# Eight buffers in place of four for the input chunks in the front of a spectral mix and FFN kernel

## What is computed

```python
X = np.fft.rfft(x, axis=1)
Yr = X.real @ w_r - X.imag @ w_i + b_r
Yi = X.real @ w_i + X.imag @ w_r + b_i
Y = soft(Yr, 0.01) + 1j * soft(Yi, 0.01)     # sign(y) * max(|y| - lam, 0)
y = np.fft.irfft(Y, n=3008, axis=1)
h = y.reshape(-1, 256) @ w_in
g = (a0 + a1*h + a2*h**2 + a3*h**3) / (1 + |b0|*|h| + |b1|*h**2 + 1e-6)
out = g @ w_out
```

## Time and profile before

| | us |
|---|---|
| median of 3 runs | 1433.96 |
| lowest and highest | 1433.38, 1437.82 |
| the profiled execution | 1435.4 |
| its span in the trace | 1433.5 |
| TensorE busy in the span | 1384.9 (97%) |
| VectorE | 1332.4 (93%) |
| ScalarE | 1249.6 (87%) |
| GpSimd | 632.1 (44%) |

### The profile page before, as it was taken

One profiled execution on the slowest core, in us unless ns is written; L12 is line 12 of the kernel. 1 busy time (PEld: TensorE's weight loads), 2 busy tenths in 40 slices (PEclk: granted clock), 3 DMA queues, 4 the chain that ended last, 5 costly groups with the idle time before them and its releaser, 6 DMA issues.

```text
span 1433.5 us, 21592 instructions
## 1 busy us (share of the span) xinstructions
PE 1384.9 (97%) x7498; PEld 972.4 (68%) x7498; DVE 1332.4 (93%) x1639; ACT 1249.6 (87%) x1654; POOL 632.1 (44%) x417
## 2 busy tenths in 40 slices
PE   7998999999999999999999999999999999999987
PEld 3775677667766677676777776776766666666666
DVE  6587989989999999999999999999999999999998
ACT  4577999988889989988989989988889999999986
POOL 0001544435444444444445444444545555555554
PEclk9999999999999999999999999999999999999999
DMA  8976756656556655555455555565445546555443
GB/s 275 293 230 140 173 129 140 154 129 140 119 130 137 143 135 131 126 115 122 105 130 114 130 108 129 110 133 115 94 103 113 117 82 122 108 114 111 85 94 70
DMA packets 97913, 188.07 MB, mean 131 GB/s; under 512 B 11216, under 2 KB 57744, under 8 KB 97808
## 3 DMA queue, kind: packets, MB, share of 16 engines
q0 software_dynamic: 29952, 98.58, 37.1%
q1 hardware_dynamic: 67856, 88.12, 20.7%
HBM read 50.60 MB, written 37.49 MB: 61 GB/s over the span
## 4 chain that ended last, share of the span: by engine, by line
PE 54%; DVE 18%; ACT 16%; issue 8%; DMA 3%; POOL 1%; SPq 0%; ACTq 0%; POOLq 0%
PE h_ps L564 19%; PE o_ps L594 7%; PE o_ps L579 6%; PE o_ps L581 6%; DVE den L1092 4%; DVE num L1098 4%; DVE g_hi L1087 4%; DVE num L1112 4%; PE d L541 3%; ACT num L794 3%; ACT sq L791 3%; ACT den L788 3%; ACT sq L857 3%; PE d L505 2%; DMA spec<-s_out 2%
## 5 line engine op out<-in xcount | busy, mean ns | idle before, releaser
L1175 POOL TENSOR_TENSOR g_lo<-num,sq 128x940 fp32r<-128x940 f32 (+1 forms) x205 | 468.8, 2287 | 97.6 <-DVE num L1098 97.0
L1167 POOL DMA_DIRECT2D den<-sq x208 | 182.5, 877 | 690.7 <-ACT sq L791 367.3
L579 PE MATMUL o_ps<-g_hi,wout_hi 128*128 128x470 f32 (+1 forms) x832 | 342.9, 413 | 2.2 <-DVE g_hi L1087 2.2
L581 PE MATMUL o_ps<-g_hi,wout_lo 128*128 128x470 f32 (+1 forms) x832 | 310.9, 374 | 0.0
L564 PE MATMUL h_ps<-yt_hi,win_hi 128*128 128x470 f16 (+1 forms) x832 | 300.8, 362 | 4.6 <-DVE num L1115 4.6
L564 PE MATMUL h_ps<-yt_lo,win_hi 128*128 128x470 f16 (+1 forms) x832 | 298.7, 359 | 0.0
L564 PE MATMUL h_ps<-yt_hi,win_lo 128*128 128x470 f16 (+1 forms) x832 | 298.7, 359 | 0.0
L1112 DVE TENSOR_TENSOR num<-h_ps,num 128x940 f32<-128x940 f32 (+1 forms) x208 | 232.3, 1117 | 31.4 <-ACT num L794 30.7
L1115 DVE SCALAR_TENSOR_TENSOR num<-num,coef,h_ps 128x940 f32<-128x940 f32 (+1 forms) x208 | 245.1, 1179 | 7.4
L1098 DVE SCALAR_TENSOR_TENSOR num<-num,a_sb,den 128x940 f32<-128x940 f32 (+1 forms) x208 | 244.4, 1175 | 0.1
L1087 DVE SCALAR_TENSOR_TENSOR g_hi<-num,a_sb,sq 128x940 fp32r<-128x940 f32 (+1 forms) x208 | 244.4, 1175 | 0.0
(11 more groups left out here) (167 smaller groups left out, 1571.7 us busy)
## 6 DMA issues: line engine op xcount, KB each, us to landing
den<-sq POOLq DMA_DIRECT2D x200, 470.0 KB, 4.4
z_in<-spec SPq DMA_DIRECT2D x96, 128.0 KB, 2.5
spec<-s_out SPq DMA_DIRECT2D x96, 128.0 KB, 1.9
xw<-in_x SPq DMA_DIRECT2D x31, 384.0 KB, 4.9
out_t<-o_sb SPq DMA_DIRECT2D x25, 470.0 KB, 4.5
spec<-s1w SPq DMA_DIRECT2D x56, 192.0 KB, 2.9
zp_in<-spec SPq DMA_DIRECT2D x22, 480.0 KB, 5.6
inv_in<-in_inv SPq DMA_DIRECT2D x96, 64.0 KB, 2.3
```

The source lines that it names most:

```text
L579: pe.matmul(o_ps[:, h, 0:w], wout_hi[:, f, h * P:(h + 1) * P], g_hi[q % 3][:, j, 0:w], start=f == 0, stop=False)
L581: mm = pe.matmul(o_ps[:, h, 0:w], wout_lo[:, f, h * P:(h + 1) * P], g_hi[q % 3][:, j, 0:w], start=False, stop=False)
L1175: pool.tensor_tensor(g_lo[r % 2][:, :, 0:cols(r)], ring(num, r), ring(sq, r), ALU.mult).then_inc(n_g, 1)
```

## The change

The chunks of x get eight buffers in the front. The four new ones are the first 96 partitions of the four num tiles. A new function x_place gives the buffer of chunk k: k % 8 for k < 10, and k % 4 from then on; x_loads counts how often a buffer was loaded, for the waits. SyncE issues chunks 4 to 7 directly after the bias, without a wait, and chunks 8 and 9 after the stores of g = 11 and g = 13 (before: 9 and 11). The load of the first four weight parts, which use num, gets two waits on all of batch 0's steps. Each buffer has its semaphore, so s_x has eight.

```diff
+def x_place(k):
+
+    return k % 8 if k < S1N // 2 + 2 else k % 4
+
+
+def x_loads(k):
+
+    return sum(1 for u in range(k + 1) if x_place(u) == x_place(k))
+
...
+        x_in += [num[i][0:ROWS, :].rearrange("r (p d) -> r p d", d=D) for i in range(4)]
...
-        s_x = [sem(f"s_x{i}") for i in range(4)]
+        s_x = [sem(f"s_x{i}") for i in range(8)]
...
             def load_x(k):
-                if k >= 4:
-                    sp.wait_ge(p1, 2 * (k - 3))
-                    if k - 3 <= FRONT_S1 // 2:
-                        sp.wait_ge(x_dve, 2 * (k - 3))
-                    else:
-                        sp.wait_ge(x_dve, FRONT_S1)
-                        sp.wait_ge(x_act, 2 * (k - 3) - FRONT_S1)
+                user = [u for u in range(k) if x_place(u) == x_place(k)]
+                if user:
+                    sp.wait_ge(p1, 2 * user[-1] + 2)
+                    sp.wait_ge(x_dve, min(2 * user[-1] + 2, FRONT_S1))
+                    if 2 * user[-1] + 2 > FRONT_S1:
+                        sp.wait_ge(x_act, 2 * user[-1] + 2 - FRONT_S1)
                 n, chunk = divmod(k, S1N // 2)
...
                 if i < 4:
+                    sp.wait_ge(p1, S1N)
+                    sp.wait_ge(x_dve, S1N)
...
-            for k in range(1, 4):
+            for k in range(1, 8):
                 load_x(k)
-            load(mix_stage(0), w_r.rearrange("(h p) e -> p h e", p=P), s_wc)
-            load(mix_stage(1), w_i.rearrange("(h p) e -> p h e", p=P), s_wc)
-            load(bias_sb[:, :], bias, s_wc)
+                if k == 3:
+                    load(mix_stage(0), w_r.rearrange("(h p) e -> p h e", p=P), s_wc)
+                    load(mix_stage(1), w_i.rearrange("(h p) e -> p h e", p=P), s_wc)
+                    load(bias_sb[:, :], bias, s_wc)
             for g in range(S1N):
                 store_s1(g)
-                if g % 2 == 1 and g // 2 + 4 < S1N // 2 + 2:
-                    load_x(g // 2 + 4)
+                if g % 2 == 1 and g // 2 + 3 in (S1N // 2, S1N // 2 + 1):
+                    load_x(g // 2 + 3)
...
-                    pe.wait_ge(s_x[g // 2 % 4], (g // 8 + 1) * 16)
+                    pe.wait_ge(s_x[x_place(g // 2)], 16 * x_loads(g // 2))
```

More of the change, by code:

```diff
@@ L325, in load_x @@
             def load_x(k):
-                if k >= 4:
-                    sp.wait_ge(p1, 2 * (k - 3))
-                    if k - 3 <= FRONT_S1 // 2:
-                        sp.wait_ge(x_dve, 2 * (k - 3))
-                    else:
-                        sp.wait_ge(x_dve, FRONT_S1)
-                        sp.wait_ge(x_act, 2 * (k - 3) - FRONT_S1)
+                user = [u for u in range(k) if x_place(u) == x_place(k)]
[4 more added lines that the diff above has]
+                        sp.wait_ge(x_act, 2 * user[-1] + 2 - FRONT_S1)
                 n, chunk = divmod(k, S1N // 2)
-                load(x_in[k % 4].rearrange("r p d -> r (p d)"), x[n, :, chunk * 4 * D:(chunk + 1) * 4 * D], s_x[k % 4])
+                load(x_in[x_place(k)].rearrange("r p d -> r (p d)"), x[n, :, chunk * 4 * D:(chunk + 1) * 4 * D], s_x[x_place(k)])
             def load_z(c):
@@ L472, in step_s1 @@
                 else:
-                    pe.wait_ge(s_x[g // 2 % 4], (g // 8 + 1) * 16)
+                    pe.wait_ge(s_x[x_place(g // 2)], 16 * x_loads(g // 2))
                 at = g % 2 * 2
-                pe.matmul(bank[0:ROWS], c1_sb[:, :], x_in[g // 2 % 4][:, at:at + 2, :].rearrange("r p d -> r (p d)"),
+                pe.matmul(bank[0:ROWS], c1_sb[:, :], x_in[x_place(g // 2)][:, at:at + 2, :].rearrange("r p d -> r (p d)"),
                           start=True, stop=True).then_inc(p1, 1)
@@ L737, in sum_abs @@
             def sum_abs(g):
-                act.wait_ge(s_x[g // 2 % 4], (g // 8 + 1) * 16)
+                act.wait_ge(s_x[x_place(g // 2)], 16 * x_loads(g // 2))
                 if g > FRONT_S1:
@@ L741, in sum_abs @@
                 at = g % 2 * 2
-                act.activation(x_size[0:ROWS, :], x_in[g // 2 % 4][:, at:at + 2, :].rearrange("r p d -> r (p d)"), ACT.Abs,
+                act.activation(x_size[0:ROWS, :], x_in[x_place(g // 2)][:, at:at + 2, :].rearrange("r p d -> r (p d)"), ACT.Abs,
                                accum_out=x_sum[0:ROWS, g:g + 1]).then_inc(x_act, 1)
@@ L886, in sum_abs @@
                 else:
-                    dve.wait_ge(s_x[g // 2 % 4], (g // 8 + 1) * 16)
+                    dve.wait_ge(s_x[x_place(g // 2)], 16 * x_loads(g // 2))
                 at = g % 2 * 2
-                dve.tensor_reduce(x_sum[0:ROWS, g:g + 1], x_in[g // 2 % 4][:, at:at + 2, :], mybir.AxisListType.XY, ALU.add,
+                dve.tensor_reduce(x_sum[0:ROWS, g:g + 1], x_in[x_place(g // 2)][:, at:at + 2, :], mybir.AxisListType.XY, ALU.add,
                                   apply_absolute_value=True).then_inc(x_dve, 1)
```

## The result

The changed kernel takes 1439.05 us (median; 1436.28 to 1441.19) against 1434.42 (1433.38 to 1437.82) of the kernel before, measured together, 11 runs of each: a ratio of 1.0030, 95% interval 1.0021 to 1.0039 (4.3 us, from 3.0 to 5.6), **4.6 us slower** by the medians. The prediction was 1434.3 us with a range to 1437.0; the time lies outside it, on the side of the rival to which I had given 17%. The span of the profiled execution is 1437.6 us, 4.1 more than before.

The account below looks back on a forecast made before the run. The prediction took a full DMA queue to bound the front: the same bytes pass, slower reads add 0.3 us to S2's start, carried 1:1 from 1433.96 to 1434.3 us; range 1431.8 to 1437.0.

Parts of the forecast that it names:

- the rival to which I had given 17%: At evacuation g = 8 the store wait grows and stalls TensorE: together +3 us, 1437.0 us; chance 17%.
- What bounds the front: From 9 to 27 us, ahead of S2: a full DMA queue at 348 to 372 GB/s, with no gap.
- The mechanism of the loss: At evacuation g = 8 ScalarE newly waits 1.8 us for the first store, which stands behind four loads.
- the rate of reads alone: Four chunks behind the bias at 348 GB/s, 1.13 us each, so the first store lands at 16.8.
- bytes conserved: Queue before S2: same bytes in another order, so the last store lands at 26.9 again, S2 +0.3 us.
- The lower bound -0.3: Four chunks read in a row at 372 GB/s would take 0.3 us less in the queue.
- queue drains: Before S2, pure reads then pure stores pass faster; S2 starts 2.1 us earlier, 1431.9 us; chance 9%.
- The waits for x: TensorE's front: at most 0.9 us beyond the first arrival; a rival had these vanish and nothing else move, 1434.0 us.
- the slower rival: Reads at 258 GB/s hold ScalarE 3.4 us at g = 8; two slow TensorE steps add 1.7; 1437.0 us, 17%.
- The carry of 1:1: From 29 us on, every step follows z in fixed order, so S2's shift reaches the end in full.
- The clock doesn't fall: Before S2, TensorE's pause is 1.3 us instead of 2.1; its clock stays up, saving 1.3 us: 1433.0; chance 15%.
- The 0.3% that I called indistinguishable: Whole kernel: about 0.3% (4.3 us) is what a measurement can tell from no change.

Follow-up runs that it names:

- e7: The kernel before with seven extra matmuls on TensorE ahead of its first step; 1435.28 us, ratio 1.0002 to the kernel before.
- e3: The changed kernel with sixteen buffers in place of eight for the results of S1; 1436.55 us, ratio 1.0013 to the kernel before.
- e5: The changed kernel with sixteen buffers for S1's results and chunks 8 and 9 back after g = 9 and 11; 1437.07 us, ratio 1.0010 to before.
- e4: The changed kernel with only chunks 8 and 9 back after the stores of g = 9 and 11; 1438.79 us, ratio 1.0025 to before.
- e6: The changed kernel with seven extra matmuls on TensorE ahead of its first step; 1440.68 us, ratio 1.0037 to the kernel before.
- e2: The changed kernel with only chunks 4 and 5 behind the bias, 6 to 9 after g = 5, 7, 9, 11; 1435.04 us, ratio 1.0000 to before.
- e8: The changed kernel with each chunk of x loaded as two DMAs with rows of 2 KB; 1440.43 us, ratio 1.0038 to the kernel before.
- e10: The changed kernel with all ten chunks of x issued ahead of the first store; 1440.74 us, ratio 1.0038 to the kernel before.
- e1: The changed kernel's eight buffers with chunks 4 to 9 issued at their old places; 1434.24 us, ratio 0.9997 to the kernel before.

## Why the prediction was wrong, point by point

*What bounds the front: right.* The DMA queue was named as the bound, and e7 shows it: 1.2 us earlier at g = 7, nothing at the end (1.0002, 0.9993 to 1.0010). One stretch, 16 to 20 us, ran at 345 GB/s, just under the 348 given as the lowest. From that full queue it doesn't follow that its time is fixed by its bytes, as the next points show.

*The mechanism of the loss: right, and put on the wrong side of the odds.* The new wait of evacuation g = 8 for the store of g = 0, its place and its reason came as described, and e3 and e5 show that it carries near half of the loss (0.0017 and 0.0015 of ratio). The sentence that on each DMA engine descriptors are consumed in ring order (the Trainium skill, "DMA: Bandwidth & Descriptors", "Queues, rings and completion order") agrees with the trace: the store, issued behind the four chunks, landed at 18.6, 0.5 us after the last of them.

*The step that failed first: the rate of reads alone.* I put a chunk at 1.13 us, from the 348 GB/s of the mixed stretch, and the first store at 16.8. From 12 to 16 us the queue ran at 258 GB/s, 393 KB / 258 = 1.52 us for a chunk, and the store landed at 18.6. I had that number in hand as the upper bound, from 4 to 9 us, and set it aside since the start of the transfers was in it; I took the 372 GB/s of 9 to 12 us for the queue's rate when full, though chunks, weights and stores pass there together. By the landing times the four chunks took 5.7 us (12.3 to 18.0), 1.44 each, against the 4.5 of the sum: 1.2 of the 1.8 us between 16.8 and 18.6 are this term, and most of the rest is the bias, which landed at 12.3 and not at 11.7 (9 to 12 us ran at 305 GB/s and not at 372). I had written that the slower case decides from 17.2 on; the rate alone put it past that point. So the prediction priced one case twice: reads at 258 GB/s are the forecast's bound of +1.6 us and the rival's +3.

*The step that failed second: bytes conserved, so the last store lands at 26.9 again.* It landed at 30.2, and S2 began 3.76 us later, not 0.3. The sum holds only while the queue stays as full and as fast. With ScalarE 3.6 us late the stores came late too, and the engines were no longer full at 24 to 29 us. For the last store I counted 1.9 us, the time of a transfer with nothing ahead of it; but chunk 9, moved behind the store of g = 13, was issued at 24.93 and stood ahead of it, and it took 3.88. Chunk 9 itself landed at 29.2, where the prediction had 26.3 and 27.0 as the latest that costs nothing. So the chunks that were moved back were not free either, though taking them forward again gives back only 0.0005 (e4), which can't be told from nothing.

*The lower bound -0.3 and the "queue drains" rival: wrong.* A run of reads isn't quicker than a mix. From the rule to issue a DMA early and wait on it late (the Trainium skill, the same page, "Rules for kernel authors") the prediction had worked out 1.9 us for the last store; it took 3.88. Here what is issued early takes its time from others in the one queue.

*The waits for x: small, right; that they would vanish, wrong.* They went from 0.9 to 1.6 us. The 0.6 us that the rival "queue drains" quotes from the earlier trace rows isn't in that row, which has 0.9; it is the difference between 23.45 and 22.9.

*The price of the slower rival: 3.0 us, measured 4.3 to 4.6.* Its first parts came: the store at 18.4 (measured 18.6), g = 15 done at 26.2 (26.3). The last store should have landed at 28.1 to 28.5 and landed at 30.2, 1.7 to 2.1 us past that. The rival had another 1.7 us for a fall of the clock, which the changed kernel's profile doesn't show before S2 (those of e4 and e6 do). One part was too small and one didn't come, so that the total is as near as it is was luck.

*The carry of 1:1: right.* +3.76 at S2, +3.9 at the first slot, +4.1 at the end. It isn't as firm as that looks: in e2's profile S2 begins 1.43 us later than before, the first slot 0.9, and the last 0.6 earlier.

*The clock doesn't fall: not borne out.* TensorE paused for 1.51 us before S2 where it had paused 2.10, and the granted clock fell after S2's start all the same (0.50 from 35 to 38 us, mean 0.81 over 32 to 41).

*The 0.3% that I called indistinguishable* was also the loss: 11 runs resolve 1.0030 from 1 by three times the half interval. The range ended at 1437.0, the rival's own price; as that price was too low, so was the end of the range.

## What to carry to other kernels

More buffers let loads be issued earlier, but in one queue each early load delays all that is issued after it. Before moving loads ahead, find the first small transfer behind them that someone waits for (here a store that frees a buffer), add up the bytes ahead of it at the rate of a stretch of the same kind (reads alone, not the mix), and compare with when it is needed: two chunks early cost nothing measurable here, four cost 0.3%. If the queue is full anyway, the waits for data are only where the queue's time shows, and more buffers don't remove them.

## What the runs showed of the hardware that I had not expected

The same DMA engines at the same busy share move different amounts by direction. Reads alone ran at 254 to 277 GB/s at a busy share of 1.03 to 1.06 (12 to 16 us in the changed kernel, e3, e4, e5, e6, e8 and e10), the mix of reads and stores at 345 to 372 GB/s (9 to 27 us in the kernel before), and stores faster still; from 20 to 24 us in e10 nearly only stores are under way:

```profile
20.00:24.00 4.00, 2.56 (x3) 0.96 (x4) 2.42 (x11) 1.58 (x3) 0.00 (x0) 0.57 1.05 401
```

Some of the spread between executions seems to be TensorE's clock: the steps 1.7 us apart ended at 14.52 in the profile of the changed kernel, at 9.57 in that of before and at 7.69 in e1's. In the body an episode at 1.2 GHz in the profile of before (granted clock 0.50 at 1000 to 1003 us) was missing from e1's (1.00 from 1000 to 1010), whose g_hi starts 0.2 us later than before at the first slot and 1.3 us earlier at the last:

```profile
L1100 DVE SCALAR_TENSOR_TENSOR g_hi<-num,a_sb,sq x208: 792/1190/1196, 129.4 to 1424.4; 128x940 fp32r<-128x940 f32 x100, 128x564 fp32r<-128x564 f32 x4
```

From its first to its last start g_hi takes 1296.5 us in the kernel before and 1295.0 in e1, so a single profile of this kernel carries about 1.5 us that have nothing to do with the change. That such episodes are the whole of it isn't shown.
